# Ninety-six unread products on TensorE between the router's rank product and the sorted rows

## What is computed

```python
logits = x @ w_gate                          # 1536 x 8
expert_idx = np.argmax(logits, axis=1)
gate_w = softmax(logits)[arange, expert_idx]
for e in range(8):
    mask = expert_idx == e
    out[mask] = gate_w[mask] * (relu(x[mask] @ w1[e]) @ w2[e])
xn = out / rms(out) * rms_g
return (silu(xn @ w_gate2) * (xn @ w_val)) @ w_out
```

## Time and profile before

| what | us |
|---|---|
| median of 3 runs | 739.77 |
| lowest and highest | 739.76 and 743.79 |
| the profiled execution | 740.22 |
| its span | 738.4 |
| TensorE busy in the span | 662.6 |

### The profile page before, as it was taken

One profiled execution on the slowest core, in us unless ns is written; L12 is line 12 of the kernel. 1 busy time (PEld: TensorE's weight loads), 2 busy tenths in 40 slices (PEclk: granted clock), 3 DMA queues, 4 the chain that ended last, 5 costly groups with the idle time before them and its releaser, 6 DMA issues.

```text
span 738.4 us, 14811 instructions
## 1 busy us (share of the span) xinstructions
PE 662.6 (90%) x6334; PEld 435.0 (59%) x6370; DVE 356.0 (48%) x621; ACT 298.1 (40%) x486; POOL 401.3 (54%) x231
## 2 busy tenths in 40 slices
PE   2899999999989229999999787999999999999995
PEld 0356666666669229999998773444444444444442
DVE  4788888888741627554546642332222222322321
ACT  1455665556644005676667824323122111121112
POOL 4476877678769582788989982524113111131112
PEclk9999999999995559999999779999999999999998
DMA  5886757665814164677868990000001000010001
GB/s 153 192 192 152 156 145 162 163 128 126 260 48 182 57 226 173 231 240 249 306 235 279 345 348 1 0 1 1 0 1 58 0 1 1 0 58 1 0 1 57
DMA packets 47073, 90.96 MB, mean 123 GB/s; under 512 B 16448, under 2 KB 20672, under 8 KB 47008
## 3 DMA queue, kind: packets, MB, share of 16 engines
q1 hardware_dynamic: 45088, 83.71, 38.7%
q0 software_dynamic: 1920, 6.31, 2.2%
HBM read 76.72 MB, written 6.30 MB: 112 GB/s over the span
## 4 chain that ended last, share of the span: by engine, by line
PE 81%; DVE 7%; POOL 5%; DMA 3%; ACT 2%; issue 2%; SPq 0%; DVEq 0%; ACTq 0%; POOLq 0%
PE psum L766 9%; PE psum L767 8%; PE psum L765 8%; PE psum L781 4%; PE psum L782 4%; PE psum L783 4%; PE psum L546 4%; PE psum L560 3%; PE psum L561 3%; PE psum L697 3%; PE psum L698 3%; PE psum L699 3%; PE psum L717 3%; PE psum L716 3%; PE psum L718 3%; PE psum L580 2%
## 5 line engine op out<-in xcount | busy, mean ns | idle before, releaser
L1237 POOL TENSOR_TENSOR low<-ring 128x4096 bf16<-128x4096 f32 x20 | 140.1, 7014 | 36.5 <-DMA ring<-in_moe_w 31.5
L1282 POOL TENSOR_TENSOR s_lo<-sv,s_hi 128x512 bf16<-128x512 f32 x36 | 41.6, 1155 | 217.1 <-ACT s_hi L803 217.1
L1217 POOL TENSOR_TENSOR probs_lo<-probs 128x768 bf16<-128x768 f32 x80 | 118.0, 1488 | 59.9 <-ACT probs L826 59.4
L826 ACT ACTIVATE probs<-psum 128x384 f32<-128x384 f32 x192 | 91.4, 490 | 68.5 <-PE psum L561 66.7
L766 PE MATMUL psum<-y,ring 128*128 128x512 bf16 x284 | 108.4, 382 | 4.7 <-DVE sv L1183 4.3
L767 PE MATMUL psum<-y,low 128*128 128x512 bf16 x282 | 107.5, 381 | 0.2
L765 PE MATMUL psum<-y,ring 128*128 128x512 bf16 x280 | 106.7, 381 | 0.3
L1176 DVE TENSOR_TENSOR gp<-psum,inv_at 128x512 f32<-128x512 f32 x36 | 24.9, 691 | 166.0 <-PE psum L767 164.8
L964 DVE TENSOR_REDUCE psum<-psum 128x1 f32<-128x768 f32 x96 | 87.7, 960 | 13.8 <-PE psum L546 13.5
L909 ACT ACTIVATE sig<-gp 128x512 f32<-128x512 f32 x36 | 22.7, 629 | 155.7 <-DVE gp L1176 155.7
L716 PE MATMUL psum<-hT,ring 128*128 128x0 bf16 x320 | 68.1, 233 | 3.5 <-POOL low L1237 3.5
(11 more groups left out here) (188 smaller groups left out, 1480.6 us busy)
## 6 DMA issues: line engine op xcount, KB each, us to landing
ring<-in_moe_w SPq DMA_DIRECT2D x20, 2048.0 KB, 8.8
pair_in<-in_qk SPq DMA_DIRECT2D x8, 768.0 KB, 4.5
head<-in_qk SPq DMA_DIRECT2D x16, 384.0 KB
head<-in_qk SPq DMA_DIRECT2D x32, 192.0 KB, 4.9
head<-pair_in SPq DMA_DIRECT2D x32, 192.0 KB, 4.0
rows_in<-sorted_x SPq DMA_DIRECT2D x12, 257.0 KB, 4.6
value<-in_v SPq DMA_DIRECT2D x16, 192.0 KB, 5.3
ring<-in_moe_w_gate SPq DMA_DIRECT2D x4, 768.0 KB, 12.5
```

What stands on the lines that cost most here:

```text
L826: nc.scalar.activation(probs[h % 2][:, t, half * HALF:(half + 1) * HALF], bank(ST_BANK + n % 2)[:, 0:HALF], ACT.Exp, scale=SCALE).then_inc ...
L1217: G.tensor_tensor(probs_lo[par][:, t, :], probs[par][:, t, :], probs_up[par][:, t, :], ALU.subtract)\
L1237: G.tensor_tensor(low[k % RING][:, :], ring[k % RING][:, :], upper[k % RING][:, :, 1], ALU.subtract)\
```

## The change

Behind the rank product TensorE waits until `ring[1]` has been loaded, and then runs 96 products: stationary `ident` (128 x 128), moving the upper halves of 512 float32 words of `ring[1]` (stride two), into bank 3. Each begins and ends its own accumulation. No semaphore is raised by them, and nothing reads their result. The wait for `table_ready` and the loads of the ten widths follow behind them.

```diff
+FILL = 96
...
             mm(bank(5)[:, 0:E * TT], tri[:, :], hot_rows, start=True, stop=True)
             mm(bank(5)[:, 128:128 + E * TT], ones[:, :], hot_rows, start=True, stop=True).then_inc(rank_ready, 1)
 
+            pe.wait_ge(w_loaded[1], 16)
+            for i in range(FILL):
+                mm(bank(3), ident[:, :], upper[1][:, 0:512, 1], start=True, stop=True)
+
 
             pe.wait_ge(table_ready, 1)
             widths = [pe.shape_register(u) for u in range(BLOCKS)]
             for u in range(BLOCKS):
                 n = pe.value_load(table[0:1, T_COUNT + u:T_COUNT + u + 1], min_val=1, max_val=WMAX)
                 pe.move_shape([widths[u]], [[(1, n)]])
```

## The result

The changed kernel takes 744.57 us (median of 18 runs, 742.70 to 750.18), the kernel before, in runs on the same chips, 741.30 us (18 runs). The ratio is 1.0036, with a 95% interval from 1.0022 to 1.0050: slower by some 2.7 us (the medians lie 3.3 us apart), well within 1%. Forecast was 741.5 against 739.77, a ratio of 1.0023, with a range of up to 749. The base of 18 runs lies 1.5 us above its first three, so the forecast is to be compared as a ratio or a shift: +1.7 us forecast, some +2.7 measured. The profiled execution has a span of 741.2 us, 2.8 more than before.

A forecast was written before the change was run, and what follows sets the result against it. VectorE's rank, GpSimd's scatter and DMAs end TensorE's gap; VectorE's copies, then TensorE, bound what follows. Span 738.4 + 2.2 (late loads) - 0.5 (clock) = 740.1, 741.9 with 1.8 around it; median 741.5, range 738.5 to 749.0.

The forecast's parts named there:

- What bounds: TensorE's gap before the first row tile (272.32): rank, scatter and DMAs set its end; later shifts pass on one for one.
- The low stretch: Start of the added products: low clock for 4.3 us (bounds 2 and 7), ten products at 0.427, then 86 at 0.225.
- The lead of the sequencer: End of the products: TensorE's sequencer runs 30 products, 6.8 us, ahead of the array; first row tile +2.2 us.
- least value: Program packets at 208.44 and 215.91: sequencer at least 45 instructions, 22 products with their weight loads, ahead of the array.
- The ten loads: Width loads behind the products: 11.1 us in all, from 263.4 to 274.5, first row tile then at about 274.5.
- The clock at the tiles: First row tiles: a clock still up gains at most 1.0 us; half taken, -0.5, bounds 0 and -1.0.
- Loads behind the products: Rival: the ten loads wait until the products are done, first row tile 9.0 us later, 748.8 us; chance 0.20.
- Sequencer far ahead: Rival: lead of 45 products or more, row tiles start as now at full clock, 738.8 us; chance 0.12.
- Clock that stays low: Rival: 96 products at 0.427 end at 287.5, row tiles 15 us late, 755 us; chance 0.04.
- Products that aren't there: Rival: unread products are absent, 739.8 us; chance 0.04, shared by nothing changes or something else.
- Everything else: Bank 3, VectorE not delayed, SBUF reads beside the scatter: no row shows such a load; ±0.3 us.
- The added wait: Ahead of the products: `ring[1]` is loaded 15 us before the wait, cost 0.

The follow-up runs named there:

- spread96: The change with its 96 products, but only block 0's width loaded ahead of the row tiles, the other nine behind hidden(0, 0) to hidden(0, 8); ratio 1.0002.
- half192: The change with 192 products of 256 columns in place of 96 of 512; 757.05 us, ratio 1.0209.
- fill128: The change with 128 products in place of 96; 751.5 us, ratio 1.0120.
- fill64_again: The change with 64 products in place of 96, run a second time; 744.14 us, ratio 1.0039.
- inter40: The kernel before with four 512-column products behind each of the ten register loads, none behind the rank; 741.31 us, ratio 1.0007.

## Why the prediction was right, and where its sizes were off

*What bounds.* Right: the products alone were hidden. They end at 270.6, before the rows land at 272.08, and the change costs only by what stands behind them in TensorE's stream. spread96 removes the loads from there and the delay of the tiles goes.

*The low stretch.* That the clock is low where the products start shows in the windows of before, 0.50 from 245 to 248 us and also under the float32 products from 222 to 245; in the change it is 0.50 until 252. The 0.427 and 0.225 us are from places at 0.50 (458 to 460 us) and at 1.00 (603 to 606). 5.9 us and fourteen products, where ten were taken; the rest at 0.222 and not 0.225. The start of the last product was forecast for about 270.0 and is 270.2. Right. But before has more than the two rises that the prediction names: one near 409.4 us, behind 3.4 us at 0.50, and one near 433.2, behind some 13.6 us at 0.50 with pauses of the array. The bounds of 2 and 7 us were an estimate of its own, and that stretch lies outside them.

*The lead of the sequencer.* This is the term that was mis-sized: 30 products, 6.8 us, taken; 18 products, 3.9 us, measured. The "least value" of 45 instructions from the packets doesn't hold behind these products, where the lead is 36. The likely error is to take the time at which a packet moves for the time at which the sequencer passes a boundary; no run tests this. It is worth 2.9 us on the slow side. The lead is about 36 in three kernels: the change, half192, and fill128 with 2.8 us between first MOVE_SHAPE and last product. Of the two places that spoke for a lead, the one on VectorE holds, but its load is shorter than the microsecond that was taken: L1128 runs from 419.6 to 420.2 us before, some 0.6 us, under the last of the L1124, which ends at 420.78.

*The ten loads.* 11.1 us taken from before; 8.2 for the last nine in the change, and the 1.2 of the first kept. Nine intervals of before hold one of 2.8 us, which the change doesn't have and fill64_again has with 3.6; what makes it is not known. This gave 1.7 us back, and the two errors partly cancel, which is luck: first tile forecast for 274.5, measured 275.77.

*The clock at the tiles.* Half of 1.0 us was taken; it was nothing, since the clock fell as the tiles began. That the low clock doubles a transpose holds: 22 in 2.47 us at 0.50 in the change, 0.112 us each, against 0.056 at 1.00. The bound of 1.0 was itself too high, as inter40 has 0.3 to 0.6: VectorE's copies could not follow each other without a break, as the third and fourth tile waited 0.47 and 0.26 us for their rows.

*Sum.* +2.2 - 0.5 = +1.7 forecast. In the profiles it is +3.4 at the first tile, with no gain from the clock, less 0.2 until the window copy and 0.4 in the last blocks: +2.8 in the span. The shift was to be passed on one for one, and it was, to 0.6 us.

*A reading.* Slices 13 to 15 of the page are 222 to 277 us, and not 240 to 295; no term of the sum uses this.

*The rivals.* Loads behind the products (748.8): refuted, four MOVE_SHAPEs run before the products' end. Sequencer far ahead (738.8): refuted by the lead of 18 products. Clock that stays low: it rose, from 0.50 to 1.00 at 252. Products that aren't there: 96 rows. *Everything else*, put at ±0.3, had a hole: no part of the prediction asked what 192 more instructions do to the delivery of the program. In this kernel they did nothing; 128 would have cost over 2 us. The added wait on `ring[1]` showed no idle time; a kernel without it was not tried.

## What to carry to other kernels

A gap on an engine's busy line is not a gap in its stream: look there for register loads, MOVE_SHAPEs and waits that print no busy time (here ten loads, 11.1 us), and add their time to what is put ahead of them. How far the sequencer got ahead of the array was here a number of instructions, about 36, so products of 512 columns hid more behind them (3.9 us) than products of 256 (2.1 us). And when a small edit costs a few microseconds at a place that it doesn't touch, look for an "issue" wait there (here 2.0 to 2.3 us) and pad the stream by a whole packet (here 256 instructions, and the wait was gone) before believing in any other cause.

## What the runs showed of the hardware

Three things that I had not expected. The delivery of TensorE's program is visible: 2.0 to 2.3 us of waiting where products start 27 ns apart, in kernels with half a packet more. Near this place no such wait shows in eight profiles of twelve, and in four it does. In half192, products of 256 columns started only once in 1.4 us for some 8 us of the scatter, while the 96 products of 512 columns ran through theirs without a gap; the cause is open. And the clock fell within a pause of 4.0 us, before work resumed (spread96, to 0.50 at 271.8), and in the change just at the end of a pause of 5.2 us (at 275.9): in both the unread products ended a few microseconds before the tiles, and the tiles had nothing of their clock.
